# Routing search on one core: where the first expert's row numbers are made, and where its tiles stand

## The chip, the cores and the metric

One NeuronCore of one Trainium2 chip. The metric is device microseconds for one launch; the median of several runs counts. The five engines run side by side, each its own instruction list in order, and meet through semaphores: TensorE (PE: matrix products into PSUM banks), VectorE (DVE), ScalarE (ACT), GpSimd (POOL, which here also issues the indirect transfers) and SyncE (SP, plain transfers).

## What is computed

A linear attention over 3072 tokens, a dense layer pair with a Mish gate, and then a layer of eight experts with a capacity of 384 tokens each. The last part is where the change lies:

```python
def _moe2_ref(x, w_gate, w1, w2):
    logits = x @ w_gate
    order = np.argsort(-logits.flatten())
    for idx in order:                      # greedy, best logit first
        tok, e = idx // E, idx % E
        if assigned[tok] >= 0 or counts[e] >= cap:
            continue
        assigned[tok] = e
        counts[e] += 1
...
    for e in range(E):
        mask = assigned == e
        h = np.maximum(x[mask] @ w1[e], 0.0)
        out[mask] = h @ w2[e]
```

## The kernel before

**Two stages.** The first stage (to about 561 us) makes the attention, the first layer pair (`tile` and `sums`, over 12 blocks of 256 tokens) and the gate logits. Its last block leaves eight output sums open, `sums(NI - 1, 0)` to `sums(NI - 1, 7)`, of 12 matrix products of 392 columns each. They feed the rows `x2` that the experts read, and not the logits, which `last_logits` makes alone.

**The search.** The greedy assignment is done as rounds r = 0, 1, ... Each round finds the next expert that fills up, and the threshold at which it does. A round is six steps t. A step is: DVE compares all keys with 32 limits (`compare`, tile `cmp`), PE counts per limit and expert (`counts`, 24 products of 8 columns), DVE reads which are full (`filled`, tile `full`), PE spreads that (`maxima`, one product), DVE takes the maximum (`most`) and sets the next limits (`next_step`). After six steps `choose` names the expert (`estar`), marks its members (`mem`), makes prefix sums (`before`), and sends the weight row numbers (`wrow`); PE makes the `ranks` from that (two products of 48 columns); DVE reads them (`take_slots`), takes the tokens out of play (`leave`), and starts the next round's search (`start_search`).

**An expert's work.** From the ranks DVE makes the row numbers: `thirds` (three small instructions), `by_third` (two), `one_hot_slot` (two halves, 1536 columns each, into `t_sb`). PE multiplies those (unit I, 24 products of 3 columns), DVE writes them as integers (`token_ids`, tile `ids`), POOL gathers the rows by three indirect transfers (`rows_in`, tile `h_sb` from `x_rows`), PE transposes them (unit X, nine), ACT and DVE split them into two halves (`g_hi`; `low_xg`), and then come eight H units (first expert layer, nine products of 384 columns) and eight Y units (second layer, the same size). ACT rounds each H tile, DVE makes the remainder (`low_h`).

**What sets the order.** The order on PE is written by hand: `PLACES` says, for each round r and each place ("A", t) between counts and maxima, ("B", t) behind the maxima, ("C", 0) behind the ranks, which units of the expert of the round before (`YOUNG` and I) or of two rounds before stand there. Round 0 has no expert's work; the sums 2 to 7 stand at its places B0 to B5 (`SUMS`). Round 1 has the first expert's I at B1, X at B4, H0 and H1 at B5, H2, Y0 and H3 at C. DVE's order is that of the loop over r, written to match. POOL's order is: weights of expert p, rows in of expert p, rows out of expert p - 1. `rows_in(0)` also waits until the rows `x2` of all blocks are stored (`x2w`); the last of them follow the last sum, through ACT (`x2s`) and ACT's own DMA queue.

Of the kernel before, what the change touches and what calls it, by code (L numbers as in the profile page):

```python
# [13 lines left out]
P = 128  # L14
# [43 lines left out]
def moe_chain(nc, wt_d, kt_d, rt_d, r_d, k_d, v_d, u_d, win_d, wout_d, wg_d, wot_d, w1_d, w2_d, out_d):  # L58
# [4 lines left out]
    with ctx:  # L63
# [208 lines left out]
        def split_out(n):  # L272
# [9 lines left out]
        YOUNG = ("X", "H0", "H1", "H2", "Y0", "H3")  # L282
        ORDER = [(c, t) for t in range(NSTEP) for c in "AB"] + [("C", 0)]


        SUMS = {("B", t): 2 + t for t in range(NSTEP)}

        def units(r, where, do):
            for u in PLACES[where]:
                p = r - 1 if u in YOUNG + ("I",) else r - 2  # L290
                if 0 <= p < E:
                    do(p, u[0], int(u[1:] or 0))
# [108 lines left out]
        def _(pe):  # L401
# [221 lines left out]
            def ranks(r):  # L623
                pe.wait_ge(s["mem"], r + 1)
                mm(R[:, 16:16 + 2 * NT], rank_b[:, :], mem[:, :], start=True, stop=False)
                mm(R[:, 16:16 + 2 * NT], ones_b[:, :], before[:, :], start=False, stop=True).then_inc(s["rank"], 1)

            def unit(p, kind, f):
# [31 lines left out]
                else:  # L660
# [11 lines left out]
                        last = mm(yb[m][:, 0:DM], lo_, wh, start=False, stop=f == F2T - 1)  # L672
                    last.then_inc(s["m2"], 1)

            for r in range(E - 1):
                for t in range(NSTEP):
                    counts(r, t)
                    units(r, ("A", t), unit)
                    maxima(r, t)
                    units(r, ("B", t), unit)  # L680
                    if r == 0:
                        sums(NI - 1, SUMS["B", t])
                ranks(r)
                units(r, ("C", 0), unit)
            ranks(E - 1)
            for r in range(E - 1, E + 2):
                for where in ORDER:
# [176 lines left out]
        def _(dve):  # L864
# [244 lines left out]
            def link(ins):  # L1109
                dve.wait_ge(s["rd"], did(ins))  # L1110
# [49 lines left out]
            def one_hot_expert():  # L1160
                V.tensor_tensor(oh[:, :, :], over_j(eighths[:, :]), over_e(pick[:, :]), ALU.is_equal
                                ).then_inc(s["oh"], 1)
# [10 lines left out]
            def filled(r, t):  # L1173
                dve.wait_ge(s["cnt"], NSTEP * r + t + 1)
                V.tensor_scalar(full[:, :], bank[6][0:NTHR, 0:E], float(CAP), None, ALU.is_ge).then_inc(s["full"], 1)
# [19 lines left out]
            def weight_row(r, x):  # L1195
                if r >= 2:
                    dve.wait_ge(w1g[r % 2], 16 * (r // 2))
                    dve.wait_ge(w2g[r % 2], 16 * (r // 2))
                V.tensor_scalar(wrow[r % 2][:, :], x, float(E * P), part_no[:, 0:1], ALU.mult, ALU.add
                                ).then_inc(s["wrow"], 1)  # L1200
# [5 lines left out]
            def choose(r):  # L1206
                t = NSTEP - 1
                dve.wait_ge(s["np"], NSTEP * r + t + 1)
                link(V.tensor_reduce(most[:, t:t + 1], bank[6][:, 8:8 + E], AX.X, ALU.max))
                m, w = most[:, t:t + 1], wid[:, t:t + 1]  # L1210
                link(V.scalar_tensor_tensor(late[:, :], bank[6][:, 8:8 + E], m, eighths[:, :], ALU.is_lt, ALU.add))
                link(V.tensor_reduce(estar[:, :], late[:, :], AX.X, ALU.min))
                did(V.tensor_scalar(above[:, :], m, w, None, ALU.mult))
                did(V.tensor_scalar(under[:, :], m, 1.0, w, ALU.subtract, ALU.mult))
                link(V.tensor_scalar(own_e[:, :], pick[:, :], estar[:, 0:1], None, ALU.is_equal))
                did(V.scalar_tensor_tensor(mem[:, 0:NT], res[:, :], above[:, 0:1], own_e[:, :], ALU.is_ge, ALU.mult))
                link(V.scalar_tensor_tensor(memlo[:, :], res[:, :], under[:, 0:1], own_e[:, :], ALU.is_ge, ALU.mult))
                link(V.tensor_tensor(mem[:, NT:2 * NT], memlo[:, :], mem[:, 0:NT], ALU.subtract))
                prefixes()
                weight_row(r, estar[:, :])  # L1220
                link(V.tensor_scalar(shut[:, :], eighths[:, :], estar[:, 0:1], OUT_OF_PLAY, ALU.is_equal, ALU.mult))
                link(V.tensor_tensor(L3, L3, over_j(shut[:, :]), ALU.add))

            def take_slots(r):
                dve.wait_ge(s["rank"], r + 1)
                link(V.tensor_reduce(slot[:, :], bank[6][:, 16:16 + 2 * NT].rearrange("p (a j) -> p j a", a=2),
                                     AX.X, ALU.min))

            def leave():
                link(V.scalar_tensor_tensor(gone[:, :], slot[:, :], -MARK + CAP, gone[:, :], ALU.is_lt, ALU.add))  # L1230

            def thirds():
                link(V.tensor_scalar(past[:, :], slot[:, :], -MARK + P, None, ALU.is_ge))
                link(V.scalar_tensor_tensor(third[:, :], slot[:, :], -MARK + 2 * P, past[:, :], ALU.is_ge, ALU.add))
                link(V.scalar_tensor_tensor(place[:, :], third[:, :], -float(P), slot[:, :], ALU.mult, ALU.add))

            def by_third():
                link(V.tensor_tensor(mine[:, :, :], over_t(third[:, :], MT),
                                     iota_m[:, :].rearrange("p (o m) -> p o m", o=1).to_broadcast([P, NT, MT]),
                                     ALU.is_equal))  # L1240
                link(V.tensor_tensor(slot_r[:, :, :], mine[:, :, :], over_t(token[:, :], MT), ALU.mult))

            def one_hot_slot(half):
                js = slice(half * NT // 2, (half + 1) * NT // 2)
                ins = V.tensor_tensor(  # L1245
                    slot_oh[:, js, :],
                    place[:, js].rearrange("p (j o) -> p j o", o=1).to_broadcast([P, NT // 2, P]),
                    iota_h[:, :].rearrange("p (o c) -> p o c", o=1).to_broadcast([P, NT // 2, P]), ALU.is_equal)
                if half == 1:
                    ins.then_inc(s["one_hot"], 1)  # L1250
# [7 lines left out]
            def low_h(p, f):  # L1258
                if not 0 <= p < E:
                    return  # L1260
                dve.wait_ge(s["hhi"], F2T * p + f + 1)
                V.scalar_tensor_tensor(h_lo[f % 3][:, :], bank[3 + f % 3][:, 0:CAP], 0.0, h_hi[f % 3][:, :],  # L1262
                                       ALU.max, ALU.subtract).then_inc(s["hlo"], 1)

            def low_xg(p):
                if not 0 <= p < E:
                    return
                for k3 in range(KT):
                    dve.wait_ge(s["xgThi"], KT * p + k3 + 1)
                    V.scalar_tensor_tensor(xgT_lo[:, k3, :], bank[3 + k3][:, 0:CAP], SX2, xgT_hi[:, k3, :],  # L1270
                                           ALU.mult, ALU.subtract).then_inc(s["xgTlo"], 1)
# [15 lines left out]

            for r in range(E - 1):
                new, old = r - 1, r - 2
                filled(r, 0)  # L1290
                low_h(old, 3)
                if r >= 1:
                    one_hot_slot(0)
                next_step(r, 0)
                if r >= 1:
                    by_third()
                filled(r, 1)
                low_h(old, 4)
                if r >= 1:
                    one_hot_slot(1)  # L1300
                next_step(r, 1)
                filled(r, 2)
                low_h(old, 5)
                next_step(r, 2)
                if r >= 1:
                    token_ids(r - 1)
                filled(r, 3)
                low_h(old, 6)
                next_step(r, 3)
                filled(r, 4)  # L1310
                low_h(old, 7)
                next_step(r, 4)
                low_xg(new)
                filled(r, 5)
                choose(r)
                pick_expert(lambda: low_h(new, 0), lambda: low_h(new, 1))
                if r < E - 2:
                    one_hot_expert()
                else:
                    weight_row(E - 1, pick[:, 0:1])  # L1320
                take_slots(r)
                leave()
                if r < E - 2:
                    start_search()
                    thirds()
                    low_h(new, 2)
# [202 lines left out]
```

## Time and profile before

| what | value |
|---|---|
| median of 3 runs | 864.26 us (863.67 to 865.05) |
| the profiled execution | 867.02 us, of which the profile's span is 865.3 us |
| PE busy | 803.1 us, 93% of the span |
| PE weight loads busy | 598.1 us, 69% |
| DVE busy | 655.6 us, 76% |
| ACT busy | 405.0 us, 47% |
| POOL busy | 290.6 us, 34% |
| granted TensorE clock over the span | 0.958 of full speed |

The page also shows the span in 40 slices of 21.6 us. In its TensorE rows all slices but a few are at 8 or 9 tenths; the hole is the slice that starts near 584 us, with 5 for products and 3 for weight loads. The granted clock's row reads 8 and 9 there and 6 in the slice behind, against 9 nearly everywhere else. So the stretch to look into is the second round of the search, from about 587 to 624 us. Times below are microseconds from the span's start. A granted clock of 1.00 is TensorE's 2.4 GHz, 0.50 is 1.2 GHz.

### The profile page before, as it was taken

The page shows a single profiled execution, that of the slowest core. Times are in us where ns is not written, and L with a number is a line of the kernel's source. Part 1 is how long each engine was busy: PE and PEld are TensorE (multiplying, and loading weights), DVE is VectorE, ACT ScalarE, POOL GpSimd, SP SyncE. Part 2 cuts the span into 40 slices and gives each one's busy share as a digit, 9 for nine tenths or more (in the row PEclk, how much of TensorE's full clock was granted, in tenths as well). Part 3 has the DMA queues.
Part 4 walks back from the last instruction along what each step waited for, and adds up shares of the span by engine and source line. Part 5 has one row for each costly group of instructions (what it writes and reads, how often), then busy time and mean ns, then how long its engine had stood idle before and what let it go on. Part 6 is the DMA issues. An engine that isn't in the chain of part 4 may idle for free.

```text
span 865.3 us, 17159 instructions
## 1 busy us (share of the span) xinstructions
PE 803.1 (93%) x6852; PEld 598.1 (69%) x6852; DVE 655.6 (76%) x1105; ACT 405.0 (47%) x655; POOL 290.6 (34%) x245
## 2 busy tenths in 40 slices
PE   7899899999999999999999999583899999999994
PEld 7789778787878787878787867352455655666662
DVE  7678988898979898979897965668668778777220
ACT  2447557575757575767666677600112211212221
POOL 3313453534343434343433450201112312313311
PEclk9699999999999999999999999896699999999998
DMA  8842236363636364545454425304414334335410
GB/s 315 315 161 77 84 101 252 109 246 119 232 134 230 136 223 144 211 155 207 160 201 153 141 98 188 141 2 170 169 29 175 114 115 175 107 123 202 182 46 28
DMA packets 47792, 133.50 MB, mean 154 GB/s; under 512 B 5345, under 2 KB 19809, under 8 KB 45665
## 3 DMA queue, kind: packets, MB, share of 16 engines
q1 hardware_dynamic: 38880, 93.07, 30.1%
q0 software_dynamic: 5376, 34.61, 10.6%
q10 hardware_dynamic: 3456, 4.72, 1.5%
q8 instruction: 55, 0.90, 0.4%
q14 instruction: 25, 0.20, 0.1%
HBM read 97.78 MB, written 34.60 MB: 153 GB/s over the span
## 4 chain that ended last, share of the span: by engine, by line
PE 54%; DVE 26%; issue 10%; DMA 4%; ACT 3%; POOL 2%; SPq 0%; DVEq 0%; ACTq 0%; POOLq 0%
PE bank L403 52%; DVE inv L880 7%; DVE cum L871 4%; DVE t_sb L957 3%; DMA h_sb<-x_rows,ids 3%; DVE h_sb L950 2%; DVE kdiv L888 2%; DVE stage L976 1%; POOL h_sb L1468 1%; DVE cmp L1165 1%; PE bank L641 1%; PE bank L427 1%; ACT t_sb L694 1%; DVE rdec L895 1%; DVE t_sb L1245 1%
## 5 line engine op out<-in xcount | busy, mean ns | idle before, releaser
L1392 POOL TENSOR_TENSOR g_lo<-t_sb,g_hi 128x512 f16<-128x512 f32 x92 | 122.1, 1346 | 120.9 <-ACT g_hi L694 120.9
L403 PE MATMUL bank<-x_hi,win_hi 128*128 128x256 f16 x576 | 159.7, 277 | 1.7 <-DVE x_lo L943 1.7
L403 PE MATMUL bank<-x_lo,win_hi 128*128 128x256 f16 x576 | 159.5, 277 | 0.0
L403 PE MATMUL bank<-x_hi,win_lo 128*128 128x256 f16 x576 | 159.5, 277 | 0.0
L403 PE MATMUL bank<-wout_hi,g_hi 128*128 128x392 f16 (+1 forms) x416 | 130.0, 319 | 8.7 <-ACT g_hi L694 7.9
L403 PE MATMUL bank<-wout_lo,g_hi 128*128 128x392 f16 (+1 forms) x416 | 130.0, 319 | 0.0
L403 PE MATMUL bank<-wout_hi,g_lo 128*128 128x392 f16 (+1 forms) x416 | 129.7, 318 | 0.0
L1376 POOL TENSOR_TENSOR dv<-v_tok,dot 128x384 f32<-128x384 f32 x24 | 39.6, 1649 | 196.1 <-DVE dot L910 196.1
L694 ACT ACTIVATE g_lo<-bank 128x384 f16<-128x384 f32 x64 | 31.4, 490 | 150.0 <-PE bank L403 127.5
L694 ACT ACTIVATE g_hi<-t_sb 128x512 f16<-128x512 f32 x96 | 57.3, 625 | 90.0 <-DVE t_sb L957 66.0
L957 DVE TENSOR_TENSOR t_sb<-t_sb,h_sb 128x512 f32<-128x512 f32 x96 | 91.4, 980 | 6.8 <-ACT t_sb L694 6.8
L694 ACT ACTIVATE t_sb<-h_sb 128x512 f32<-128x512 f32 x96 | 60.1, 626 | 67.9 <-DVE h_sb L950 67.8
L880 DVE RECIPROCAL inv<-cum 128x256 f32<-128x256 f32 x48 | 83.3, 1737 | 0.0
L950 DVE TENSOR_SCALAR h_sb<-bank 128x512 f32<-128x512 f32 x96 | 64.0, 667 | 18.1 <-PE bank L403 18.0
L694 ACT ACTIVATE t_sb<-t_sb,half 128x512 f32<-128x512 f32 x96 | 66.8, 706 | 0.0
L403 PEld LDWEIGHTS bank<-x_hi,win_hi 128*128 128x128 f16 x576 | 57.7, 100 | 11.1 <-issue 2.1
L403 PEld LDWEIGHTS bank<-wout_hi,g_hi 128*128 128x128 f16 x416 | 40.8, 100 | 33.1 <-ACT g_hi L694 8.0
L1468 POOL DMA_INDIRECT h_sb<-x_rows,ids x24 | 26.3, 1094 | 110.7 <-DVE ids L1256 105.9
L403 PEld LDWEIGHTS bank<-x_lo,win_hi 128*128 128x128 f16 x576 | 57.2, 99 | 7.7
L403 PEld LDWEIGHTS bank<-x_hi,win_lo 128*128 128x128 f16 x576 | 57.3, 99 | 7.5
L1262 DVE SCALAR_TENSOR_TENSOR g_lo<-bank,g_lo 128x384 f16<-128x384 f32 x64 | 35.1, 548 | 36.0 <-ACT g_lo L694 28.5
L976 DVE SCALAR_TENSOR_TENSOR stage<-stage 128x1536 f16<-128x1536 f32 x32 | 56.0, 1750 | 7.7 <-ACT stage L694 7.4
(165 smaller groups left out, 1557.4 us busy)
## 6 DMA issues: line engine op xcount, KB each, us to landing
stage<-in_moe_w SPq DMA_DIRECT2D x32, 768.0 KB, 6.7
w_split<-stage SPq DMA_DIRECT2D x32, 768.0 KB, 5.4
wt<-in_w_turned SPq DMA_DIRECT2D x24, 258.0 KB, 5.0
kt<-in_k_turned SPq DMA_DIRECT2D x24, 256.0 KB, 4.5
rt<-in_r_turned SPq DMA_DIRECT2D x24, 256.0 KB, 5.5
r_tok<-in_r SPq DMA_DIRECT2D x24, 192.0 KB, 6.4
k_tok<-in_k SPq DMA_DIRECT2D x24, 192.0 KB, 7.0
v_tok<-in_v SPq DMA_DIRECT2D x24, 192.0 KB, 4.9
```

The source lines that it names most:

```text
L403: return nc.tensor.matmul(*a, **k)
L694: return nc.scalar.activation(out, in_, f, **k)
L871: V.tensor_tensor_scan(cum[n % CH][:, :, :].rearrange("p q t -> p (q t)"), wt[n % CH][:, :, :].rearrange("p q t -> p (q t)"), heads[:, :, ...
L880: V.reciprocal(inv[:, qs, :], cum[n % CH][:, qs, 1:PW]).then_inc(s["inv"], 1)
L888: V.tensor_tensor(kdiv[n % CH][:, :, :], kt[n % CH][:, :, :], inv[:, :, :], ALU.mult).then_inc(s["kdiv"], 1)
L950: V.tensor_scalar(h_sb[:, j * GW:(j + 1) * GW], hb[HB[j]][:, :], 0.5, None, ALU.mult).then_inc(s["hcp"], 1)
L957: V.tensor_tensor(t, t, h_sb[:, j * GW:(j + 1) * GW], ALU.mult).then_inc(s["g"], 1)
L976: V.scalar_tensor_tensor(out[:, 1, :], split_raw(n), (SW1, SW2)[n // 2 % 2], out[:, 0, :], ALU.mult, ALU.subtract).then_inc(s["plo"], 1)
L1262: V.scalar_tensor_tensor(h_lo[f % 3][:, :], bank[3 + f % 3][:, 0:CAP], 0.0, h_hi[f % 3][:, :], ALU.max, ALU.subtract).then_inc(s["hlo"], 1)
L1376: G.tensor_tensor(dv[:, :, :], v_tok[c][:, :, :], dot[:, :].rearrange("p (h o) -> p h o", o=1).to_broadcast([P, H, D]), ALU.mult).then_inc ...
L1392: G.tensor_tensor(g_lo[:, j * GW:(j + 1) * GW], t_sb[:, j * GW:(j + 1) * GW], g_hi[:, j * GW:(j + 1) * GW], ALU.subtract).then_inc(s["glo" ...
L1468: G.indirect_dma_start(xg[m][:, :], None, x2_d, bass.IndirectOffsetOnAxis(ap=ids[p % 3][:, m:m + 1], axis=0)).then_inc(s["xg"], 16)
```

## The change

Three things change, all around rounds 0 and 1.

- `SUMS` ends two places earlier: the last two sums of the first stage (`sums(NI - 1, 6)` and `sums(NI - 1, 7)`) leave B4 and B5 of round 0 and stand behind the ranks of round 0. Behind them stand 8 products of the identity with itself that nothing reads (`idle_products`), then unit I of the first expert, then 12 more such products.
- On DVE the row numbers of the first expert (`take_slots`, `thirds`, `by_third`, both `one_hot_slot`) are made inside `choose(0)`, behind the prefix sums and ahead of the update of the logits; the search of round 1 starts after them. `token_ids(0)` follows its first comparison.
- Round 1 has its own places: X at B1, H0 at B2, H1 at B3, H2 at B4, Y0 at B5, H3 at C. DVE's part of round 1 is written out for it.

```diff
+        PLACES_1 = {("B", 1): ["X"], ("B", 2): ["H0"], ("B", 3): ["H1"], ("B", 4): ["H2"], ("B", 5): ["Y0"],
+                    ("C", 0): ["H3"]}
...
-        SUMS = {("B", t): 2 + t for t in range(NSTEP)}
+        SUMS = {("B", t): 2 + t for t in range(NSTEP - 2)}
...
-            for u in PLACES[where]:
+            for u in (PLACES_1 if r == 1 else PLACES).get(where, []):
...
+            def idle_products(n):
+                for _ in range(n):
+                    mm(bank[3][:, 0:P], ident[:, :], ident[:, :], start=True, stop=True)
...
-                    if r == 0:
+                    if r == 0 and ("B", t) in SUMS:
                         sums(NI - 1, SUMS["B", t])
                 ranks(r)
                 units(r, ("C", 0), unit)
+                if r == 0:
+                    for j in (NJ - 2, NJ - 1):
+                        sums(NI - 1, j)
+                    idle_products(8)
+                    unit(0, "I", 0)
+                    idle_products(12)
...
                 weight_row(r, estar[:, :])
+                if r == 0:
+                    take_slots(0)
+                    thirds()
+                    by_third()
+                    one_hot_slot(0)
+                    one_hot_slot(1)
...
+                if r == 1:
+                    for t in range(NSTEP):
+                        filled(r, t)
+                        if t == 2:
+                            low_xg(new)
+                        elif t > 2:
+                            low_h(new, t - 3)
+                        if t < NSTEP - 1:
+                            next_step(r, t)
+                    choose(r)
+                    pick_expert()
+                    one_hot_expert()
+                    take_slots(r)
+                    leave()
+                    start_search()
+                    thirds()
+                    continue
...
-                take_slots(r)
+                if r >= 1:
+                    take_slots(r)
                 leave()
-                if r < E - 2:
+                if r == 0:
+                    start_search()
+                    token_ids(0)
+                elif r < E - 2:
```

In the rows below `bank<-wout_hi,g_hi` and its two neighbours are products of a sum, `oh,cmp` the counts, `full` the maxima, `mem` and `before` the ranks, `slot_r,t_sb` unit I, `ident,h_sb` unit X, `g_hi,win_hi` and `win_lo,g_lo` H units and halves of Y units, `bank<-ident` alone the unread products.

PE from the fifth count of round 0 to the ranks, before:

```order
L403 MATMUL bank<-oh,cmp 32x8 x24
L403 MATMUL bank<-full,rest_b 128x8
L403 MATMUL bank<-wout_hi,g_hi 128x392
...
L403 MATMUL bank<-wout_hi,g_lo 128x392
L403 MATMUL bank<-mem,rank_b 128x48
L403 MATMUL bank<-before,ones_b 128x48
```

and in the changed kernel, from the fifth count on:

```order
L406 MATMUL bank<-oh,cmp 32x8 x24
L406 MATMUL bank<-full,rest_b 128x8
L406 MATMUL bank<-oh,cmp 32x8 x24
L406 MATMUL bank<-full,ones_b 128x8
L406 MATMUL bank<-mem,rank_b 128x48
L406 MATMUL bank<-before,ones_b 128x48
...
L406 MATMUL bank<-wout_hi,g_lo 128x392
L406 MATMUL bank<-ident 128x128 x8
L406 MATMUL bank<-slot_r,t_sb 128x3 x24
L406 MATMUL bank<-ident 128x128 x12
```

The 24 products of two sums moved from in front of the ranks to behind them, with the 20 unread products and unit I.

PE in round 1 before, from its fourth count to the ranks:

```order
L403 MATMUL bank<-oh,cmp 32x8 x24
L403 MATMUL bank<-full,rest_b 128x8
L403 MATMUL bank<-oh,cmp 32x8 x24
L403 MATMUL bank<-full,rest_b 128x8
L641 MATMUL bank<-ident,h_sb 128x128 x9
L403 MATMUL bank<-oh,cmp 32x8 x24
L403 MATMUL bank<-full,ones_b 128x8
L403 MATMUL bank<-g_hi,win_hi 128x384 x18
L403 MATMUL bank<-mem,rank_b 128x48
```

and in the changed kernel, from its second count:

```order
L406 MATMUL bank<-oh,cmp 32x8 x24
L406 MATMUL bank<-full,rest_b 128x8
L644 MATMUL bank<-ident,h_sb 128x128 x9
L406 MATMUL bank<-oh,cmp 32x8 x24
L406 MATMUL bank<-full,rest_b 128x8
L406 MATMUL bank<-g_hi,win_hi 128x384 x9
L406 MATMUL bank<-oh,cmp 32x8 x24
L406 MATMUL bank<-full,rest_b 128x8
L406 MATMUL bank<-g_hi,win_hi 128x384 x9
L406 MATMUL bank<-oh,cmp 32x8 x24
```

The transposes moved up by three steps, and three H units that stood together behind the last step now stand one each behind the third, fourth and fifth.

DVE behind the prefix sums of round 0, in the changed kernel:

```order
L1245 TENSOR_REDUCE slot<-bank 128x24
L1252 TENSOR_SCALAR past<-slot 128x24
L1253 SCALAR_TENSOR_TENSOR third<-slot,past 128x24
L1254 SCALAR_TENSOR_TENSOR place<-third,slot 128x24
L1257 TENSOR_TENSOR mine<-third,iota_m 128x72
L1260 TENSOR_TENSOR slot_r<-mine,token 128x72
L1264 TENSOR_TENSOR t_sb<-place,iota_h 128x1536 x2
L1240 TENSOR_SCALAR shut<-eighths,estar 128x8
```

These seven rows stood behind or inside the search of round 1 and now stand ahead of its first comparison.

## Rows read from the trace of the kernel before

**Rows 1.** Timeline of PE, 585 to 624 us: start, duration, instruction, idle before.

```profile
585.07 0.34 PE L403 MATMUL bank<-wout_hi,g_hi 128*128 128x392 f16 x1
...
586.90 0.33 PE L403 MATMUL bank<-wout_hi,g_lo 128*128 128x392 f16 x1
587.31 0.20 PE L403 MATMUL bank<-mem,rank_b 128*128 128x48 bf16 x1
...
591.54 0.77 PE L403 MATMUL bank<-oh,cmp 128*32 128x8 bf16 x24 [4.02 <-DVE cmp L1165]
...
598.45 0.80 PE L403 MATMUL bank<-slot_r,t_sb 128*128 128x3 f16 x24 [1.48 <-DVE t_sb L1245]
...
609.94 2.18 PE L641 MATMUL bank<-ident,h_sb 128*128 128x128 f32 x9 [3.15 <-DMA h_sb<-x_rows,ids]
612.05 0.80 PE L403 MATMUL bank<-oh,cmp 128*32 128x8 bf16 x24
...
613.47 5.83 PE L403 MATMUL bank<-g_hi,win_hi 128*128 128x384 f16 x18
...
620.65 1.63 PE L403 MATMUL bank<-win_lo,g_lo 128*128 128x384 f16 x9
...
623.67 0.76 PE L403 MATMUL bank<-oh,cmp 128*32 128x8 bf16 x24
```

**Rows 2.** Timeline of DVE, 585 to 646 us.

```profile
585.17 0.17 DVE L1209 TENSOR_REDUCE most<-bank 128x1 f32<-128x8 f32 x1 [0.27 <-PE bank L403]
...
587.27 0.22 DVE L1221 TENSOR_SCALAR shut<-eighths,estar 128x8 f32<-128x8 f32 x1
...
590.44 0.96 DVE L1165 TENSOR_TENSOR cmp<-key,first 128x768 bf16<-128x768 f32 x1
591.32 0.17 DVE L1233 TENSOR_SCALAR past<-slot 128x24 f32<-128x24 f32 x1
...
592.50 1.73 DVE L1245 TENSOR_TENSOR t_sb<-place,iota_h 128x1536 f16<-128x1536 f16 x1
...
596.03 0.23 DVE L1238 TENSOR_TENSOR mine<-third,iota_m 128x72 f32<-128x72 f32 x1
...
601.62 0.96 DVE L1165 TENSOR_TENSOR cmp<-key,thr 128x768 bf16<-128x768 f32 x1
...
604.40 0.96 DVE L1165 TENSOR_TENSOR cmp<-key,thr 128x768 bf16<-128x768 f32 x1
...
621.73 0.96 DVE L1165 TENSOR_TENSOR cmp<-key,first 128x768 bf16<-128x768 f32 x1
...
645.53 1.49 DVE L1270 SCALAR_TENSOR_TENSOR g_hi<-bank,g_hi 128x384 f16<-128x384 f32 x3 [0.67 <-ACT g_hi L694]
```

**Rows 3.** Stretches: length, PE busy (records), granted clock, DMA share, GB/s.

```profile
8.20:11.00 2.80, 2.80 (x27) 1.00 0.91 332
561.00:564.40 3.40, 3.40 (x12) 0.50 0.01 2
587.50:591.70 4.20, 0.18 (x9) 1.00 0.57 170
...
609.90:619.00 9.10, 8.56 (x52) 0.50 0.16 34
619.10:623.60 4.50, 4.50 (x30) 1.00 1.00 421
```

**Rows 4.** Timelines of ACT and of POOL, 585 to 612 us.

```profile
587.26 0.87 ACT L694 ACTIVATE x2s<-bank 128x384 f32<-128x384 f32 x2 [26.09 <-PE bank L403]
...
603.45 0.95 POOL L1468 DMA_INDIRECT h_sb<-x_rows,ids  x1 [12.63 <-DVE ids L1256]
```

**Rows 5.** The chain that ended last, two transfers in it: start, duration, what.

```profile
587.78 1.85 DMA x_rows<-x2s
...
606.49 3.41 DMA h_sb<-x_rows,ids
```

**Rows 6.** All 24 stores to `x_rows`: time from issue to landing.

```profile
DMA to landing us min/median/max: 1.8/2.8/4.3
```

## Prediction, made before the changed kernel ran

> **What bounds the kernel now.** I read the summary of busy shares first: PE is busy for 93% of the span, and the one hole in its 40 slices starts near 584 us. So the question is what the change makes of that hole, and I read PE's timeline through it. The ranks of the first round start at 587.31; from there to 609.94 PE has only counts, maxima and unit I, each behind a wait; the transposes X start at 609.94 on a transfer, the counts behind them at 612.05, 18 products of H at 613.47, and the counts of the third round at 623.67 [rows 1]. From 623.67 on the changed program has the same order on every engine, and PE is nearly always busy, so I take the time of these counts as the measure: whatever they move by, the end moves by. DVE's timeline shows the other half: the comparison that opens the second search starts at 590.44 and the one that opens the third at 621.73; a step of the search with nothing in it but the search takes 2.78 us (601.62 to 604.40) [rows 2]. The third view is the granted clock by stretches: 1.00 until the hole, 0.50 in the busy stretch from 609.9 to 619.0, and 1.00 again behind it [rows 3]. The H units of the first expert therefore run at 1.2 GHz: 18 products in 5.83 us, 0.324 us each, against 0.162 at the full clock (nine in 1.46, from the 1.63 of a row less the 0.17 that its last product takes to drain) [rows 1].
>
> **DVE behind the first ranks.** In place of the update of the logits, DVE first waits for the ranks (587.31, read some 0.2 later: 587.5). Then come the slots (0.2), three small steps and two more at 0.17 to 0.23 each plus about 0.04 between dependent ones (1.2 together), and two halves of the one-hot at 1.7 [rows 2]. It ends at 592.4. From `shut` to the first comparison it took 3.17 us (587.27 to 590.44), less 0.24 for the slots that are already read: 2.93. The comparison of the second search starts at 595.3, 4.9 later than before. The same instructions leave the steps of that search, which then take the bare 2.78. So on DVE alone this edit costs about 2 us (4.9 less the part of the two one-hot halves that was not hidden in two steps).
>
> **The two sums.** Before, they stand beside DVE's work at places that waited anyway, so taking them out of round 0 gives back at most 0.3 us: the sixth counts follow directly behind a sum. I count 0.25. Behind the ranks they need 24 products of 0.166 us at full clock (585.07 to 586.90 is eleven of them) [rows 1], 4.0 us, or 8.0 at half. Which clock? Without them PE has about 6 us, from the end of the fourth step's sum to the ranks, with only 8-column counts and single products. In the row of 587.5 to 591.7 PE did nothing but a few counts and the stretch behind it stood at 0.50 when X came; a dense run of 3.40 us at 561.0 was still at 0.50 [rows 3]. So I expect a fall to 0.50 before the ranks and a return some 3.7 us into the sums (the sum products of that row had begun only just before it). That makes 11 products at 0.33 and 13 at 0.166: 5.8 us, from 587.5 to 593.3. At the ends it is 4.0 and 8.0; I take 5.8 because that row is the same kind of product after the same kind of gap.
>
> **The unread products and unit I.** An identity product is two records, at 0.107 us each at full clock (27 records in 2.80 us) [rows 3], so 8 cost 1.7 and 12 cost 2.6. They were to fill a wait: the one-hot is ready at 592.4, but PE comes to unit I only at 595.0. Unit I takes 0.8 [rows 1], and 12 more end at 598.4. The first comparison was ready at 596.3. So the first counts of the second search start 2.1 us after they could. A comparison and the counts behind it stand 1.1 apart (590.44 and 591.54) [rows 1, 2], so the search runs as if its comparison had started at 597.4; its third comparison starts at 603.0 (two bare steps).
>
> **The stores and the gather.** `x2s` follows the last sum: 587.26 before, 593.4 now. A store is issued 0.5 later (587.26 to 587.78) and the second some 0.4 behind it, since the two copies ahead of them take 0.87 together [rows 4, 5]. Before, the first landed in 1.85 us, ahead of the expert's weights. Now these are under way. The 24 stores of the kernel took 1.8 to 4.3, in the median 2.8 [rows 5, 6]. I take 2.8, which puts the last landing at 597.2. The row numbers are written by 596.5 (behind the comparison that starts at 595.3 and takes 0.96), so the stores decide. The gather starts at 597.4, and from the first gather to X it took 6.5 us (603.45 to 609.94) [rows 1, 4], of which 3.41 is the last transfer [rows 5]. X starts at 603.9. With the third counts queued behind it on PE, a late X stops the search.
> The Trainium skill ("DMA: Bandwidth & Descriptors", "Issuing engines are not separate DMA queues") says that transfers issued by ACT and by POOL run on the same 16 DMA engines and interleave. That speaks for the 2.8 rather than the 1.85; with 1.85 X would start at 603.0 and the sum would be 0.9 less. The trace before has no such pair side by side at this place.
>
> **The tiles between the steps.** X takes 2.1 us at half clock to the counts behind it [rows 1]: 606.0. The counts are read 0.85 later, 606.85. `low_xg` takes 1.5 [rows 2]: 608.35. H0 waits for it and runs at half clock, 2.9 us, to 611.3; the fourth counts are queued behind it, although their comparison (started at 608.85) was ready at 609.8. From there a step is no longer the 2.78 of DVE but PE's own: counts 0.85, maxima 0.3, an H unit 2.9, together 4.05. Counts are read at 612.15, 616.2 and 620.3. `low_h` adds 0.5 before the maximum (620.8), from which the first round took 5.27 to the comparison of the next (585.17 to 590.44) [rows 2]: 626.1. The third search's counts stand 1.1 behind, 627.2, against 623.67. Y0 and H3 (5.8 at half clock) fit between 620.6 and 627.2. The sum is +3.5, less the 0.25 of above: +3.25.
>
> Why half clock for the H units: between the unread products (598.4) and X (603.9) PE has two counts of 8 columns and little else, the same filling as the stretch that fell [rows 3]; and each H unit now has a gap of 1.1 us behind it, where before 609.9 to 619.0 was busy for 8.56 of 9.10 us and came back only at its end [rows 3].
> The Trainium skill ("TensorE: Matmul & The Clock Gate", "HAM oscillation — how this bites in real kernels") advises to run tiles together before the next wait, since bursts with waits between them each run at the low clock; it speaks against spreading H0 to H2. By that rule the result is the sum above; without it, it is the first rival.
>
> **Rivals.**
> (a) *The clock holds or is back at once*, and the change is faster. The sums then take 4.0, the row numbers rather than the stores decide the gather (596.6), X starts at 603.1 and takes half, 1.05; counts read at 605.0, `low_xg` 606.5, next comparison 607.0; three DVE-bound steps of 2.9 bring the last reading to 614.7, the third search's comparison to 620.5, its counts to 621.6: -2.1, with the 0.25 some -2.3. For it: the 20 unread products do keep PE dense from 587.5 to 598.4. Against it: the 5 us behind them.
> (b) *The clock comes back during H0 or H1.* Each H unit at full clock is 1.46 shorter, and a step is then 2.9, so 1.15 less each; two of them give 2.3, and +1.0 is left: within what can be told from nothing. For it: an H unit of 2.9 us is as long a dense piece as any that brought it back.
> (c) *The stores land at 4.3 and the clock stays low into the third round.* The first gives +1.5; the second makes Y1 and H4 1.46 longer each, of which some is idle time now: +1. Together about +5.7.
> (d) *The first gain fails.* That the row numbers are not ready earlier at all can be excluded: one-hot at 592.4 against 598.4 before (unit I started at 598.45) [rows 1].
> The deciding point between (a) and the forecast is the time that PE needs for an H unit: below 1.7 us the step is DVE's, above it PE's.
>
> **How the numbers follow.** The profiled execution took 867.02, with a span of 865.3; the median of the runs is 864.26. The sum is a difference against that execution's span, and I carry it to the median: 864.26 + 3.25 = 867.5. Before's own return of the clock, 5.6 us after H began, may be earlier or later in another run, by some 1 us on that side; it goes into the range. Chances: the forecast 0.57 (865.9 to 869.0), (a) 0.15 (862.0), (b) 0.18 (865.2), (c) 0.10 (up to 870). The range leaves out most of (a) and the far end of (c): 862.6 to 869.6. A difference under 0.2%, 1.7 us, can't be told from no change with this kernel; faster by more than that is (a) but for a little, 0.14; within it is (b) with a rest of (a) and of the forecast, 0.19; slower 0.67.
>
> **What would show it.** In the changed profile: the granted clock at 0.50 from before the ranks until some 3 to 5 us into the sums; the last sum near 593; unit I at 595, the second search's first counts near 598.4 with PE and not DVE as what they waited for; X near 604 behind a transfer; three steps of 4.05 with nine products in 2.9; the third search's counts near 627. If the H rows read 1.6 for nine, (a) or (b) is right. If X comes before 603, the stores were not late. If the distance from the third search's counts to the end is not 241.6, as before (865.3 - 623.67), my measure is wrong.

## The result, and the profile after

The changed kernel is slower. In the first timing it took 873.62 us in the median of 4 runs (870.1 to 877.17) against 863.96 for the kernel before (861.71 to 865.05): ratio 1.0112, 95% interval 1.0082 to 1.0141. Ten more runs, beside 33 of before, gave 871.73 against 864.86: 1.0074, interval 1.0051 to 1.0097. The forecast was slower by 3.25 us; the loss is 7 to 10. Two single runs, at a lower granted clock than the other runs of their kernels, are left out of the ratios below: one of the kernel before (874.26 us, at 0.908) and one of e5 (1189 us, at 0.643).

The span of the profiled execution is 868.4 us, against 865.3. That comparison says little by itself: both kernels scatter by 3 to 9 us from run to run (before: 859.33 to 868.02 in 33 runs), part of it in the first stage, where the change has nothing. In the changed profile the first ranks start at 584.64, in the one before at 587.31 [rows 1]. So below I measure from the first ranks to the counts that open the third search, and call this distance **D**. Before, D was 36.4 us (587.31 to 623.67 [rows 1]); behind it 241.6 us remain. In the changed profile D is 43.2 and 240.5 remain: +6.9 in the stretch, nothing lost behind it. In a second profile of the changed kernel D is 43.1.

PE's timeline of the changed kernel, from the first ranks to the third search (start, duration, instruction, idle before). Its rows answer to [rows 1]:

```profile
584.64 0.22 PE L406 MATMUL bank<-mem,rank_b 128*128 128x48 bf16 x1 [2.17 <-DVE before L1216]
...
591.48 1.95 PE L406 MATMUL bank<-ident 128*128 128x128 f32 x16
593.27 0.75 PE L406 MATMUL bank<-slot_r,t_sb 128*128 128x3 f16 x24
593.88 2.92 PE L406 MATMUL bank<-ident 128*128 128x128 f32 x24
596.74 0.76 PE L406 MATMUL bank<-oh,cmp 128*32 128x8 bf16 x24
...
599.45 0.76 PE L406 MATMUL bank<-oh,cmp 128*32 128x8 bf16 x24 [1.54 <-DVE cmp L1178]
...
605.14 2.18 PE L644 MATMUL bank<-ident,h_sb 128*128 128x128 f32 x9 [4.43 <-DMA h_sb<-x_rows,ids]
607.25 0.81 PE L406 MATMUL bank<-oh,cmp 128*32 128x8 bf16 x24
...
609.82 3.04 PE L406 MATMUL bank<-g_hi,win_hi 128*128 128x384 f16 x9 [1.25 <-issue]
...
614.03 3.06 PE L406 MATMUL bank<-g_hi,win_hi 128*128 128x384 f16 x9
...
618.25 1.64 PE L406 MATMUL bank<-g_hi,win_hi 128*128 128x384 f16 x9
...
627.86 0.78 PE L406 MATMUL bank<-oh,cmp 128*32 128x8 bf16 x24 [2.53 <-DVE cmp L1178]
628.58 2.98 PE L406 MATMUL bank<-win_lo,g_lo 128*128 128x384 f16 x9
```

The longest idle time is the 4.43 us ahead of X at 605.14; the counts behind it come at 607.25, while their comparison started at 601.23. What X waits for is in the chain of waits of the same kernel (start, duration, what):

```profile
592.59 6.18 DMA x_rows<-x2s
...
599.53 0.73 POOL h_sb L1508
...
602.04 3.06 DMA h_sb<-x_rows,ids
```

This is the second of the last two stores, 192 KB each, and it took 6.18 us; before, the first of the two took 1.85 [rows 5], and the longest of 24 took 4.3 [rows 6]. POOL's gather is released by it and not by the row numbers (594.06 on DVE, 5.5 us earlier):

```profile
599.53 0.94 POOL L1508 DMA_INDIRECT h_sb<-x_rows,ids  x1 [10.57 <-DMA x_rows<-x2s]
```

The stretches in the changed kernel (length, PE busy, granted clock, DMA share, GB/s), to stand beside [rows 3]:

```profile
577.00:583.00 6.00, 3.13 (x59) 1.00 0.01 3
583.70:590.30 6.60, 5.66 (x20) 0.50 0.38 134
590.50:600.50 10.00, 7.92 (x120) 1.00 0.71 258
600.70:617.60 16.90, 10.57 (x99) 0.50 0.13 36
617.80:627.80 10.00, 6.01 (x56) 1.00 0.20 54
628.00:631.30 3.30, 3.30 (x33) 0.50 1.01 428
```

The clock is at 1.2 GHz for most of the two sums and again from before X to the end of H1, where nine products take 3.04 and 3.06 us; H2 has 1.64. Behind the third search's first counts it is low once more: the first half of a Y unit takes 2.98 us there.

### The profile page after: what moved, and what is told of

Its sections match the earlier page's. It is cut to its first block, busy times and chain, and to the rows that moved or that the text cites. A ratio compares the mean times of both kernels' runs of the same rounds, so it can differ in the third digit from the quotient of the medians.

```text
span 868.4 us, 17236 instructions
## 1 busy us (share of the span) xinstructions
PE 809.4 (93%) x6892; PEld 600.5 (69%) x6892; DVE 653.8 (75%) x1105; ACT 404.9 (47%) x655; POOL 291.0 (34%) x245
## 4 chain that ended last, share of the span: by engine, by line
PE 51%; DVE 29%; issue 9%; DMA 4%; ACT 3%; POOL 2%; SPq 0%; DVEq 0%; ACTq 0%; POOLq 0%
PE bank L406 48%; DVE inv L893 7%; DVE cum L884 4%; DVE t_sb L970 3%; DMA h_sb<-x_rows,ids 2%; DVE h_sb L963 2%; DVE cmp L1178 2%; DVE kdiv L901 2%; DVE stage L989 1%; POOL h_sb L1508 1%; PE bank L644 1%; PE bank L430 1%; ACT t_sb L707 1%; DVE g_lo L1281 1%; DVE rdec L908 1%
## 5 line engine op out<-in xcount | busy, mean ns | idle before, releaser
L406 PEld LDWEIGHTS bank<-x_hi,win_hi 128*128 128x128 f16 x576 | 57.9, 100 | 11.3 <-issue 2.2
L1508 POOL DMA_INDIRECT h_sb<-x_rows,ids x24 | 25.8, 1074 | 104.6 <-DVE ids L1275 89.1
L707 ACT ACTIVATE t_sb<-t_sb,half_pi 128x512 f32<-128x512 f32 x96 | 60.7, 709 | 0.1
```

Source lines behind the costliest of these rows:

```text
L406: return nc.tensor.matmul(*a, **k)
L707: return nc.scalar.activation(out, in_, f, **k)
L1508: G.indirect_dma_start(xg[m][:, :], None, x2_d, bass.IndirectOffsetOnAxis(ap=ids[p % 3][:, m:m + 1], axis=0)).then_inc(s["xg"], 16)
```

## The experiments

Theory A: the loss is the late X, and X is late because the stores of the last rows are issued into the transfer of the expert's weights. Theory B: the loss is TensorE's low clock under the sums, X and the H units. Both are about the same 43 us, so nearly every run takes away one of them alone. The runs are called a0 and e1 to e10. D is from one profile each; the ratios are against the kernel before on the same chip, and are not the quotients of the medians, from which they differ by up to 0.2%.

**The changed kernel again (a0).**

> The changed kernel unaltered, for a second profile. In its first profile the third search's counts stand 43.2 us behind the first ranks (627.86 less 584.64), before 36.4 (623.67 less 587.31): +6.9. Theory A (the stores of the last rows, issued at 592.2 into the transfer of the expert's weights, land 6 us later, and X waits for them): the distance is 43 again within 1.5, in every profile, and the time 6 to 7 us over before. Theory B (TensorE's clock, which falls and comes back at other places from run to run, makes the large difference between the runs of 870.1 and 877.2): the distance is over 45 in a slow run, with H0 to H2 all at nine products in 3.0 us and a first Y and H of the third round at the low clock.

Ratio 1.0074 (1.0051 to 1.0097), D 43.1. Its runs went from 869.35 to 874.39. What sets the upper end of these is not shown to lie in this stretch: in this profile the first ranks are 2.9 us later than in the first one, and D is the same. The store took longer still, and X started 21.7 us behind the ranks in place of 20.5. The row is from its chain of waits:

```profile
594.15 8.34 DMA x_rows<-x2s
```

But H1 was already at the full clock, where the first profile has 3.06 us for it:

```profile
618.15 1.64 PE L406 MATMUL bank<-g_hi,win_hi 128*128 128x384 f16 x9
```

So the stretch loses the same by two different roads, a later X and a shorter H1, and a D over 45, which theory B would have needed for the long times, did not show.

**The last two sums back in front of the ranks (e2).**

```diff
-        SUMS = {("B", t): 2 + t for t in range(NSTEP - 2)}
+        SUMS = {("B", t): 2 + t for t in range(NSTEP)}
...
-                    for j in (NJ - 2, NJ - 1):
-                        sums(NI - 1, j)
```

> The last two sums back in front of the ranks, at B4 and B5 of the first round; all else as in the changed kernel. The stores are then issued near the ranks, ahead of the weights. Theory A: they land within 2 to 3 us, the row numbers decide the gather, X starts some 15.5 us behind the ranks in place of 20.5, and the third counts stand 38 us behind them: 5 us less than in the changed kernel, about 868.5. Theory B: the clock also stays up to the ranks; the unread products keep it up to the second search, but X and the H units still come at the low clock, since PE has little between the first two counts and X; no more than the 5 us is gained.

Ratio 1.0036 (1.0006 to 1.0065), median 866.79, D 39.1 where 38 was said. The stores land 2.3 and 2.8 us behind the ranks, the gather starts at 9.3 and X at 15.2. PE reaches X without a wait, but at the low clock:

```profile
589.20 2.03 PE L406 MATMUL bank<-ident 128*128 128x128 f32 x16
594.37 0.80 PE L406 MATMUL bank<-slot_r,t_sb 128*128 128x3 f16 x24 [3.15 <-DVE t_sb L1262]
595.04 5.47 PE L406 MATMUL bank<-ident 128*128 128x128 f32 x24
...
604.38 2.18 PE L644 MATMUL bank<-ident,h_sb 128*128 128x128 f32 x9
```

The 12 unread products behind unit I took 5.47 us here, since the wait ahead of it let the clock fall, and held the first counts to 11.3 us behind the ranks. X came 5.3 us earlier than in the changed kernel, but H2 was at the low clock too (3.06 us in place of 1.64), so theory A's 5 us became 4.1. What is left over the kernel before, 2.7 in D, is not the stores.

**The gather ahead of the weights on GpSimd (e3).**

```diff
             for p in range(E):
-                weights(p)
-                rows_in(p)
+                if p == 0:
+                    rows_in(p)
+                    weights(p)
+                else:
+                    weights(p)
+                    rows_in(p)
```

> Changed kernel with one edit on GpSimd: for the first expert the gather of its rows is issued ahead of its weights, not behind them, so that neither the stores nor the gather meet the weights. Sums, unread products and tiles stay where they are. Theory A: the stores land within 3 us of their issue at 592.2, the gather starts near 595, X near 600.6 in place of 605.1, the third counts 4.5 us earlier: about 869. The weights come 7 us later, to about 606, ahead of H0. Theory B: X earlier, but H0 to H2 at the low clock as before. If the stores still land 6 us late, theory A is wrong.

Ratio 1.0036 (1.0004 to 1.0069), median 868.89, D 37.8. Sums, unread products and tiles stand as in the change, the weights alone are out of the way, and the last store, issued near 594.8 (0.4 behind the first of 594.42), has landed by 596.75, 2 us later, so that the row numbers release the gather. X starts 15.9 us behind the ranks in place of 20.5. D falls by 5.4 although the weights now are the late ones (H0 waits 1.82 us for them). Not all of this is the stores: X is 4.6 earlier, and the rest came because H1 was at the full clock here (1.64 us in place of 3.06). In time this version is 2.8 us under the changed kernel (868.89 against 871.73), less than D says and hardly clear of the scatter. The wait of H0:

```profile
608.87 3.04 PE L406 MATMUL bank<-g_hi,win_hi 128*128 128x384 f16 x9 [1.82 <-DMA win_hi<-w_split,wrow]
```

That the stores were late because of the weights is shown: with the weights behind them they took 1.9 us, and with the weights ahead 6.2 and 8.3.

**The tiles back at their old places (e4).** X again behind the fifth step, H0 and H1 behind the sixth; DVE's part of the second round is moved back to match, which the diff here leaves out.

```diff
-        PLACES_1 = {("B", 1): ["X"], ("B", 2): ["H0"], ("B", 3): ["H1"], ("B", 4): ["H2"], ("B", 5): ["Y0"],
-                    ("C", 0): ["H3"]}
+        PLACES_1 = {("B", 4): ["X"], ("B", 5): ["H0", "H1"], ("C", 0): ["H2", "Y0", "H3"]}
```

> Changed kernel with the tiles of the first expert where they were (X behind the fifth step, H0 and H1 behind the sixth, H2, Y0, H3 behind the ranks); row numbers, sums and unread products as changed. Theory A: a gather that lands at 605 holds nothing up, since X stands behind the fifth maxima at about 609; counts of the sixth step near 611, third counts near 622.6, 5 us less than in the changed kernel: about 868.5. If spreading the tiles is what the change gains by, this is slower than the changed kernel by some 2 us instead.

Ratio 1.0002 (0.9973 to 1.0031), median 863.71, D 36.0. The stores are as late as ever (landed 13.5 and 14.0 us behind the ranks) and cost nothing: PE comes to X only at 23.3 us and does not wait for it. D is 2 us less than was said, half of it because X came at 23.3 and not at some 24.4, half because H0 and H1 took 4.85 us together and not 5.8, the clock having come back under them. So neither the late stores nor the place of X makes the loss of 6.9 by itself; it takes the two together.

**Unread products in the changed kernel's waits (e6).** 6, 20 and 5 more of them, behind the first, second and third maxima of the second round (into another PSUM bank).

```diff
+            FILL = (6, 20, 5, 0, 0, 0)
...
                     maxima(r, t)
+                    if r == 1:
+                        idle_products(FILL[t], 2)
                     units(r, ("B", t), unit)
```

> Changed kernel with unread products also in the second round: 6 behind the first maxima, 20 behind the second (ahead of X), 5 behind the third (ahead of H0). They only keep TensorE busy while it waits. Theory B (the low clock in X, H0 and H1 is a part of the loss by itself): the clock stays at 1.00 from the sums to the third round, X takes 1.1 in place of 2.1, nine products 1.5 in place of 3.0, and the distance D from the first ranks to the third counts falls from 43.2 to about 39: 4 us less. Theory A alone (only the late stores count): X still starts 20.5 us behind the ranks, and D falls by 1 at most.

Ratio 1.0040 (1.0007 to 1.0073), D 39.3. X starts 20.4 us behind the ranks, no earlier than before, and everything from there is at 2.4 GHz:

```profile
606.25 1.20 PE L644 MATMUL bank<-ident,h_sb 128*128 128x128 f32 x9 [1.09 <-DMA h_sb<-x_rows,ids]
...
609.90 1.62 PE L406 MATMUL bank<-g_hi,win_hi 128*128 128x384 f16 x9
...
612.63 1.64 PE L406 MATMUL bank<-g_hi,win_hi 128*128 128x384 f16 x9
```

From X to the third search the clock is worth 3.9 us in the changed kernel, as theory B had it (39). Both theories hold: late stores put X back by 4.6 us (e3), the low clock costs 3.9. Together that is more than the 6.9 lost, because the change has gains too, which the two hide: with both out of the way, and its tiles one place later, e10 below is 4.2 us under the kernel before in D.

**Unread products in the kernel before (e5).** 18 behind the ranks, and `FILL = (12, 6, 6, 6, 14, 0)`.

> The kernel before with unread products in the waits of the second round: 18 behind the first ranks, then 12, 6, 6, 6 and 14 behind the maxima of its first five steps. Theory B: the clock does not fall at 591.8 any more, X takes 1.2, H0 and H1 together 2.9 in place of 5.8, and D falls from 36.4 to about 33: 3 to 3.5 us less, near 861. If the clock matters little there, nothing changes; if the unread products themselves delay the counts, it is slower by up to 2 us.

Ratio 1.0004 (0.9980 to 1.0028), D 36.0: no gain. The profile shows a wait that the edit does not account for: in the fifth step DVE stood still for 2.2 us, though its counts were done at 608.1, and the profile names no engine of this core for it:

```profile
609.88 0.15 DVE L1185 TENSOR_SCALAR full<-bank 32x8 bf16<-32x8 f32 x1 [2.21 <-remote]
```

TensorE was idle with it, the clock fell from 611.6 to 615.0, and 14 unread products ahead of X took 5.0 us, where 12 had taken 2.94. X started at 25.8 and not at 22.6; nine products then had 1.5. What stopped DVE stays open, and so does why nothing was gained: the eleven runs behind the ratio have one profile between them, and whether the others had such a wait no trace shows. So the 3.5 us that theory B gave this kernel are not confirmed.

**Early row numbers alone (e7).** Sums as before, no unread products, tiles at their old places; unit I behind the ranks. DVE's part of the second round is as in e4.

> Only the early row numbers of the change, with unit I behind the ranks: sums back at B4 and B5 of the first round, no unread products, tiles where they were. DVE starts the second search 4.6 us later than before, and its first two steps are bare: the counts of the sixth step, which in both kernels wait behind X, are free of that wait now, since X can start at once behind the fifth maxima. By my sum for DVE (2 us lost by moving the work, 3.5 won by a gather that no longer ends the wait): D about 35, 1.5 us less than before. If the transfer was never what mattered, D is 38.

D 34.9, as said; ratio 1.0004 (0.9980 to 1.0028), so 1.5 us in D is not told from nothing in the time. That D agrees is luck. The forecast wanted the gain from an earlier X, and X starts 22.6 us behind the ranks in both kernels: without a wait now, but the search ahead of it is later by as much. The 1.4 us come from the clock, which came back sooner under H0 and H1 (5.83 us before):

```profile
615.52 4.43 PE L405 MATMUL bank<-g_hi,win_hi 128*128 128x384 f16 x18
```

So the first part of the change neither loses nor, by itself, is shown to gain.

**The two sums moved, alone, in the kernel before (e8).**

> The kernel before with one part of the change alone: the last two sums behind the first ranks. The stores then meet the weights and land some 13 to 14 us behind the ranks, but the gather waits for the row numbers until 16 anyway. The sums run at the low clock at first, 6 to 7 us, and delay the first counts by 2 to 3 us. Theory A says D rises by those 2 to 3 and by nothing for the stores: 38 to 39. If the late stores cost something by themselves, D is over 40.

Ratio 1.0021 (0.9996 to 1.0046), D 38.3. The first counts come 6.9 us behind the ranks and not 4.2; the stores land after 13.4 and 13.9 and nobody waits, since the row numbers come at 18.6. The sums put X back by 2.5 us, of which a clock that came back sooner under H0 and H1 returned 0.6; the late stores by themselves cost nothing. This measures the second part of the change.

**The changed kernel without its unread products (e1).**

> Changed kernel without its 20 unread products. The first counts of the second search then start when their comparison is ready, 9 us behind the ranks in place of 11 to 12, but X still waits for the late stores until 20.5 to 21.7: D stays at 43 within 1, and the time at that of the changed kernel. If the unread products were what the loss is made of, D falls by 2 to 3.

Ratio 1.0088 (1.0065 to 1.0112), D 42.8. The first counts start at 9.1, 3 us earlier than in the changed profile; 6.99 us of idle time stand ahead of X in place of 4.43, and nothing is gained. The 20 products neither were the loss nor kept the clock to X.

**A version that is faster: early row numbers, filled waits (e9).** From e7, with 21 and 13 unread products around unit I and `FILL = (6, 6, 6, 6, 0, 0)`.

> The early row numbers alone (as in e7: D was 34.9, before 36.4), with unread products that fill TensorE's waits: 21 behind the first ranks ahead of unit I, 13 behind it, 6 behind each of the maxima of the second round's first four steps. Theory A and B together: the stores are early, the gather is early, the clock stays at 1.00, X takes 1.2 and nine products 1.5, and D is about 33.3, 3 us less than before: 0.35%, near 862. If D falls and the time does not, something outside of this stretch pays for the unread products.

Ratio 0.9962 (0.9939 to 0.9984), median 862.02 against 864.83. D is 32.2. The whole stretch is at the full clock (first line), X is not waited for and starts 1.3 us earlier than before (21.3 us behind the ranks in place of 22.6), and H0 and H1 together take 3.1 us where they took 5.83 [rows 1]. The two make up nearly all of the 4.2 us in D:

```profile
589.00:621.00 32.00, 28.81 (x348) 1.00 0.44 162
```

```profile
610.25 1.20 PE L643 MATMUL bank<-ident,h_sb 128*128 128x128 f32 x9
...
613.66 3.10 PE L405 MATMUL bank<-g_hi,win_hi 128*128 128x384 f16 x18
```

**The same with the tiles spread, one place later (e10).** X behind the third step, H0, H1, H2 behind the fourth to the sixth, `FILL = (6, 6, 0, 5, 0, 0)`.

> As e9, with the tiles between the steps as in the change, but one place later (X behind the third step, H0, H1, H2 behind the fourth to the sixth, Y0 and H3 behind the ranks), where the gathered rows are there before X is reached. If spreading the tiles is sound once nothing makes X late and the clock is up, D is at or under that of e9, 33 to 33.6; if the tiles between the steps hold the search up by themselves, D is 35 or more.

Ratio 0.9966 (0.9937 to 0.9996), median 861.08, D 32.2. Spread tiles cost nothing once X finds its rows and the clock is up, and gain nothing in D either over tiles that stand together.

## Why the prediction was right in its way and wrong in its size

Times here are from the first ranks on; the prediction's own are less 587.31.

| step | forecast | measured |
|---|---|---|
| one-hot ready | 5.1 | 5.2 |
| last sum done | 6.0 | 6.8 |
| unit I | 7.7 | 8.6 |
| first counts of the second search | 11.1 | 12.1 |
| second store landed | 9.9 | 14.1 |
| first gather issued | 10.1 | 14.9 |
| X | 16.6 | 20.5 |
| third search's counts (D) | 39.9 | 43.2 |

The hole that I started from is where I said, but its digits are misread: 5, 3 and 8 belong to the slice near 541 us. The one near 584 us has 3 for products, 2 for weight loads and 6 for the granted clock. Nothing in the sum used them.

- **DVE behind the ranks**: right to 0.1.
- **The clock under the sums**: right. It fell before the ranks and was back 5.7 us into them, where I had taken 3.7 from the nearer of two rows; 1 us on the first counts, which X hid again. In the second profile it was back after 2.9 us and the first counts came at 10.7, with the same D.
- **The unread products**: right in their price (1.8 and 2.9 against 1.7 and 2.6) and in their use, none, as e1 showed.
- **The stores: the step that failed.** I took 2.8 us to land and gave 1.85 and 4.3 as its ends, from the 24 stores of the kernel before. It was 6.2 and 8.3. None of those 24 had met an indirect transfer of weights: 22 lay in the first stage, where the other transfers are SyncE's, and the last two were issued at 587.8 and 588.2, ahead of the weights. So my bounds were from another neighbour, and I had written down that no such pair was there, without widening for it. The term was short by 3.4 to 5.5 us (1.85 to 4.3 on offer, 6.18 to 8.34 measured). Of the 3.9 us by which X came later than forecast in the first profile, 3.4 are this term and 0.9 the slower sums; the gather started 0.6 later behind the landing and needed 0.9 less to X. e3 shows the same stores at 2 us with the weights away, and X is back at 15.9. What I should have priced is the end of the weights: in the changed kernel's two profiles and in e4 and e8 the first store was issued 6.2 to 7.6 us behind the ranks, and in all four the second landed at 13.9 to 14.9, whichever was issued sooner.
- **X holds the search up**: right in its kind, and this is why the missing microseconds all came through. From X to the third counts the forecast was 23.3 and it took 22.7: H0 and H1 at 3.0 where 2.9 was said, while H2 had the full clock.
- **D to time**: the end lies 240.5 us behind the third counts, before 241.6; the measure held for the change. In the variants it holds within some 2 us only: e3 is 1.5 over before in D and e2 2.7, and both have the ratio 1.0036, which is 3.1 us. D says +6.9, the second timing +6.9, the first +9.7 with four runs.

Rival (a), the clock held, did not come; its price for X, H0 and H1 did, in e6 (3.9 us). Rival (b) came for H2 alone in the first profile, for H1 and H2 in the second; its reason, that no longer piece than an H unit had brought the clock back, does not fit the rows that I had (3.40 dense us were still at 0.50 [rows 3]). Rival (c) is the nearest and had 0.10. It named late stores, at 4.3, and they went beyond it (6.2 and 8.3); and it named a low clock in the third round, where one half of a Y unit did take 2.98 us, though the end behind the third counts was no later for it.

## What to carry to other kernels

Where a change moves a transfer, look up what else is on the queues at its new time, and price it by a row with that same neighbour; if there is none, put the upper bound just behind the end of the neighbour's transfer, where these stores landed. An instruction that can wait on a transfer should not stand in front of a short serial chain on an engine that runs in order: the same late rows cost 7 us behind the second step and nothing behind the fifth. Filling TensorE's waits pays where real products follow at once and what is filled ends before its wait does; here it was worth 4 us in the changed kernel, and with the early row numbers it made the version that beat both. In the kernel before no gain was found (e5), and 12 unread products that came after a wait, at the low clock, held the search up instead (e2).

## What the runs showed of the hardware that I had not expected

**A store behind the weights' transfer waited for nearly all of it.** While the weights come, the DMA engines are full; then comes the store's turn (stretches of the changed kernel: length, busy of PE, PE loads, DVE, ACT, POOL, clock, DMA share, GB/s):

```profile
592.20:596.00 3.80, 3.80 (x55) 3.79 (x54) 1.50 (x5) 0.36 (x1) 0.00 (x0) 1.00 1.02 346
596.00:598.80 2.80, 1.67 (x33) 1.36 (x31) 0.93 (x4) 0.00 (x0) 0.00 (x0) 1.00 0.55 208
```

The queues show whose bytes these are: q0 has the indirect transfers, q10 the stores (packets, MB, share of 16 engines). In the first stretch q0 is the only one, in the second both are there:

```profile
q0 software_dynamic: 114, 1.31, 102.3%
...
q10 hardware_dynamic: 288, 0.39, 37.8%
q0 software_dynamic: 30, 0.17, 14.7%
```

The stores, issued at 592.2 and 592.6, landed at 598.3 and 598.8; the last of the weights, issued at 587.2, took 10.7 and landed at 597.9. In the second profile the weights landed at 601.9 and the stores at 602.1 and 602.5. Beside SyncE's loads of the first stage, at lower rates (187 GB/s from 217.2 to 221.9 in the kernel before), the kernel's stores took at most 4.3. The Trainium skill ("DMA: Bandwidth & Descriptors", "Issuing engines are not separate DMA queues") says that transfers of all issuing engines interleave; of the change's stores and weights the measurement shows no sharing for 3.8 us and then only at the weights' end. Why, no run here shows.

**The clock after a filled wait.** Products of the identity hold it: 28.81 us of PE busy in 32.00 stood at 1.00 throughout, with the counts of 8 columns among them. X at the full clock took 1.20 in place of 2.18, transposes as they are.
